# Reciprocals of the softmax through a table in DRAM instead of transposes: one fused attention and mixture-of-experts kernel

## The reference

```
B, H, S, D = 2, 8, 1152, 64
q_pool = q.reshape(B, H, S // 2, 2, D).mean(axis=3)            # 576 queries a head
scores = scale * q_pool @ k^T                                    # 576 x 1152
attn   = exp(scores - max(scores))
attn   = attn / (sum(attn) + 1e-9)                               # row by row
x      = attn @ v                                                # 576 x 64 a head
```

## Time and profile before

| | |
|---|---|
| median of 3 runs | 892.01 us |
| lowest and highest | 891.36, 893.62 us |
| the profiled execution | 892.18 us |
| its span | 890.2 us |
| mean granted clock of PE | 0.969 |
| attention, pairs 0 to 7 | about 20 to 270 us of the span |

### The profile page before, as it was taken

One profiled execution on the slowest core, in us unless ns is written; L12 is line 12 of the kernel. 1 busy time (PEld: TensorE's weight loads), 2 busy tenths in 40 slices (PEclk: granted clock), 3 DMA queues, 4 the chain that ended last, 5 costly groups with the idle time before them and its releaser, 6 DMA issues.

```text
span 890.2 us, 13115 instructions
## 1 busy us (share of the span) xinstructions
PE 837.6 (94%) x4706; PEld 714.4 (80%) x4707; DVE 397.0 (45%) x644; ACT 311.2 (35%) x509; POOL 218.1 (24%) x186
## 2 busy tenths in 40 slices
PE   6899999999999999999999999999996089999996
PEld 6787878788779898898989998898985078878885
DVE  3676766767575323421414223421414212796235
ACT  2565645556443211220303111220315012675233
POOL 4845955775631000000000000000000400232012
PEclk7999999999999999999999999999997579999998
DMA  7843425243263202200202002200000631596310
GB/s 186 266 112 93 107 68 134 67 111 90 70 183 120 71 1 95 95 1 1 94 1 94 0 0 94 95 1 1 1 1 0 226 105 47 192 331 227 144 42 19
DMA packets 30105, 79.83 MB, mean 90 GB/s; under 512 B 4007, under 2 KB 4007, under 8 KB 30064
## 3 DMA queue, kind: packets, MB, share of 16 engines
q1 hardware_dynamic: 26944, 69.99, 25.4%
q0 software_dynamic: 2960, 8.68, 2.8%
q10 hardware_dynamic: 160, 0.59, 0.3%
HBM read 69.52 MB, written 10.78 MB: 90 GB/s over the span
## 4 chain that ended last, share of the span: by engine, by line
PE 87%; DMA 4%; DVE 3%; POOL 2%; issue 2%; ACT 1%; SPq 0%; ACTq 0%; POOLq 0%; DVEq 0%
PE L L472 23%; PE L L415 22%; PE ring L388 8%; PE scores L353 8%; PE L L587 8%; PE L L561 7%; PE ring L367 6%; DMA rawQ<-in_qT 1%; DMA xr<-sorted_rows 1%; PE scores L376 1%; DVE negmax L785 1%; POOL sorted_rows L1146 1%; PE L L569 1%; ACT a L618 1%; DMA out<-o,destc 1%
## 5 line engine op out<-in xcount | busy, mean ns | idle before, releaser
L415 PE MATMUL L<-xTh,w1h 128*128 128x384 f32 x384 | 128.5, 335 | 0.0
L415 PE MATMUL L<-xTh,w1l 128*128 128x384 f32 x384 | 128.4, 334 | 0.0
L415 PE MATMUL L<-xTl,w1h 128*128 128x384 f32 x384 | 128.3, 334 | 0.0
L656 ACT ACTIVATE hh<-L 128x384 fp32r<-128x384 f32 x96 | 46.6, 491 | 201.3 <-PE L L415 201.3
L472 PE MATMUL L<-w2h,hh 128*128 128x512 f32 x288 | 114.3, 397 | 0.0
L472 PE MATMUL L<-w2h,hl 128*128 128x512 f32 x288 | 113.8, 395 | 0.0
L472 PE MATMUL L<-w2l,hh 128*128 128x512 f32 x288 | 113.7, 395 | 0.0
L1146 POOL DMA_INDIRECT sorted_rows<-acc,posi x9 | 10.7, 1188 | 414.3 <-DVE posi L976 411.9
L884 DVE SCALAR_TENSOR_TENSOR hl<-L,hh 128x384 fp32r<-128x384 f32 x96 | 52.9, 557 | 123.7 <-ACT hh L656 123.3
L618 ACT ACTIVATE a<-scores,negmax 128x1152 f32<-128x1152 f32 x72 | 88.0, 1222 | 39.6 <-DVE negmax L785 39.6
L785 DVE TENSOR_REDUCE negmax<-scores 128x1 f32<-128x1152 f32 x72 | 97.2, 1350 | 5.0 <-PE scores L353 4.8
(11 more groups left out here) (171 smaller groups left out, 1357.4 us busy)
## 6 DMA issues: line engine op xcount, KB each, us to landing
raw<-in_v SPq DMA_DIRECT2D x48, 512.0 KB, 5.5
raw<-in_w SPq DMA_DIRECT2D x32, 512.0 KB, 5.3
rawK<-in_kT SPq DMA_DIRECT2D x32, 288.0 KB, 4.5
rawQ<-in_qT SPq DMA_DIRECT2D x30, 288.0 KB, 5.7
sorted_rows<-filler SPq DMA_DIRECT2D x19, 257.0 KB, 5.7
V<-in_vr SPq DMA_DIRECT2D x16, 288.0 KB, 3.1
xr<-sorted_rows POOLq DMA_DIRECT2D x15, 257.0 KB
rawQ<-in_qT ACTq DMA_DIRECT2D x2, 288.0 KB, 6.1
```

The costliest lines, as they stand in the source:

```text
L415: last = pe.matmul(L1[i % L1_BANKS][:, 0:CW], w[:, d, wf], x[:, cols], start=(n == 0), stop=(n == 3 * DT - 1))
L656: act.activation(hh[c % 2][:, f, :], L1[i % L1_BANKS][:, 0:CW], ACT.Relu) \
```

## The change

PE no longer turns the reciprocals, and GpSimd no longer spreads them. SP does it by DMA (`share_rinv`): it waits for the reciprocals of a pair, stores the 128 x 9 numbers to a table `reciprocals` in DRAM, ordered by tile and query, waits until they have landed, and loads them back in three pieces, each row of queries repeated over 64 partitions, to a new tile `nb` of 128 x 576 in SBUF. The multiplication `y = o * nb` is one operation. In pairs 0 to 6 GpSimd does it, ahead of its split of the same pair: it prepares one of the next heads, multiplies and splits, and then prepares the other. In the last pair DVE does it. SyncE's share for pair j stands in its program between the loads for heads 2j + 4 and those for heads 2j + 5, and the last one ahead of the filler stores.

```diff
+            def share_rinv(j):
+                sp.wait_ge(S["rinv_ready"], j + 1)
+                sp.dma_start(recip[j].rearrange("(t p) -> p t", p=P), rinv[:].rearrange("p a t -> p (a t)")[:, 0:TPP],
+                             allow_slow_non_contiguous=True).then_inc(S["rinv_out"], 16)
+                sp.wait_ge(S["rinv_out"], 16 * (j + 1))
+                at_least(sp, S["y_ready"], j)
+                sp.dma_start(nb[0:DH, :], recip[j, 0:QS].partition_broadcast(DH)).then_inc(S["nb_in"], 16)
+                sp.dma_start(nb[DH:P, FULL * P:], recip[j, QS:QS + XW].partition_broadcast(DH)).then_inc(S["nb_in"], 16)
+                sp.dma_start(nb[DH:P, 0:FULL * P], recip[j, QS + XW:].partition_broadcast(DH)).then_inc(S["nb_in"], 16)
...
                 if n + 2 < NH:
                     load_kq(n + 2, n % 2)
+                if n % 2 == 0:
+                    share_rinv(n // 2 - 1)
+            share_rinv(PAIRS - 1)
...
                 if ahead:
                     score_part(g + LEAD, range(SC))
-                    spread_rinv(g, 0)
-                    spread_rinv(g, 2)
...
             times_v(PAIRS - 1, 1)
-            pe.wait_ge(S["spread_ready"], 2 * PAIRS)
-            for t in range(FULL):
-                last = pe.transpose(L2[1][:, t * P:(t + 1) * P], spread[:, t * P:(t + 1) * P], ident[:])
-            last.then_inc(S["nb_ready"], N_DONE - 1)
-            pe.transpose(L2[0][:, 0:P], spread[:, FULL * P:], ident[:]).then_inc(S["nb_ready"], 1)
...
                 if s == 0:
-                    at_least(act, S["y_ready"], Y_DONE * j)
+                    at_least(act, S["y_ready"], j)
...
                     take_last(g - 1)
-                    if spread_blocks(g - 1):
-                        normalize(g - 1)
...
+            dve.wait_ge(S["nb_in"], 48 * PAIRS)
+            dve.wait_ge(S["x_lo"], PAIRS - 1)
+            tt_(y[:], o[:], nb[:], ALU.mult).then_inc(S["y_ready"], 1)
...
             def split_x(j):
-                pool.wait_ge(S["y_ready"], Y_DONE * (j + 1))
+                pool.wait_ge(S["o_low"], v_done(j, 1))
+                pool.wait_ge(S["o_high"], v_done(j, 1))
+                pool.wait_ge(S["nb_in"], 48 * (j + 1))
+                at_least(pool, S["x_lo"], j)
+                pool.tensor_tensor(y[:], o[:], nb[:], ALU.mult).then_inc(S["y_ready"], 1)
+                pool.wait_ge(S["y_ready"], j + 1)
...
             for j in range(PAIRS):
-                if j:
-                    spread_pair(j - 1)
...
-            spread_pair(PAIRS - 1)
```

More of the change, by code:

```diff
@@ L29 @@
 V_STEP = (5, TPP)
-N_STEP = {2: ((0, 0), (1, 2)), 3: ((2, 0), (3, 2)), 4: ((FULL, 0),)}
 WARM = 23
-Y_DONE = 4
-N_DONE = sum(len(blocks) for blocks in N_STEP.values())
 SC = 3
@@ L56, with attention_moe_moe_kernel @@
 NEPS = 1e-6
-def attention_moe_moe_kernel(nc, kT, qT, vr, dom, w1, w2, emb, tau, v1, v2, rows, out):
+def attention_moe_moe_kernel(nc, kT, qT, vr, dom, w1, w2, emb, tau, v1, v2, rows, recip, out):
     ctx = ExitStack()
@@ L122, in attention_moe_moe_kernel @@
         totale = sb("totale", [P, TPP + 1], F32, att)
-        spread = sb("spread", [P, (FULL + 1) * P], F32, att)
+        nb = sb("nb", [P, QS], F32, att)
         rinv = sb("rinv", [P, 2, FULL + 1], F32, att)
@@ L248, in last_view @@
             return halved(g % TPP, spare(g + LEAD, 1).rearrange("p (i q) -> p i q", q=P))
-        def spread_blocks(g):
-            j, k = g // TPP, g % TPP
-            return N_STEP[k] if j and k in N_STEP else ()
         names = """consts_in kq_in0 kq_in1 v_in0 v_in1 k_hi k_lo q_sum q_scaled q_hi q_lo s_ready max_ready
-            exp_ready den_ready rinv_ready t_ready0 t_ready1 t_ready2 nb_ready a_out0 a_out1 a_out2 o_ready o_low o_high spread_ready y_ready pads_ready emb_in
+            exp_ready den_ready rinv_ready t_ready0 t_ready1 t_ready2 nb_in a_out0 a_out1 a_out2 o_ready o_low o_high rinv_out y_ready pads_ready emb_in
             x_hi x_lo w1_hi w1_lo w2_hi w2_lo l1_ready h_hi l1_free l2_ready l2_free
@@ L391, in times_v @@
                 last.then_inc(S["o_ready"], 1)
[L393 to L399, removed]
             def up_tile(e, c, f):
@@ L800, in take_o @@
                 if s == 0:
-                    at_least(dve, S["y_ready"], Y_DONE * j)
+                    at_least(dve, S["y_ready"], j)
                 dve.tensor_copy(o[s * DH:(s + 1) * DH, HALF:QS], bank(("V", j, s))[DH:P, 0:HALF]) \
@@ L811, in rinv_pair @@
                     .then_inc(S["rinv_ready"], 1)
[L813 to L838, removed]
             dve.wait_ge(S["kq_in0"], 64)
@@ L868, in _ @@
             take_o(PAIRS - 1, 1)
[L869 to L873, removed]
+            dve.wait_ge(S["o_low"], NH)
+            dve.wait_ge(S["o_high"], NH)
+            dve.wait_ge(S["nb_in"], 48 * PAIRS)
+            dve.wait_ge(S["x_lo"], PAIRS - 1)
+            tt_(y[:], o[:], nb[:], ALU.mult).then_inc(S["y_ready"], 1)
             last_cols = slice((PAIRS - 1) * QS, PAIRS * QS)
-            dve.wait_ge(S["y_ready"], Y_DONE * PAIRS)
+            dve.wait_ge(S["y_ready"], PAIRS)
             dve.tensor_copy(xTh[:, last_cols], y[:]).then_inc(S["x_hi"], 1)
@@ L1075, in prep_q @@
                     .then_inc(S["q_lo"], 1)
[L1077 to L1084, removed]
-            def split_x(j):
-                pool.wait_ge(S["y_ready"], Y_DONE * (j + 1))
+            def split_x(j):
+                pool.wait_ge(S["o_low"], v_done(j, 1))
[4 more added lines that the diff above has]
+                pool.wait_ge(S["y_ready"], j + 1)
                 cols = slice(j * QS, (j + 1) * QS)
@@ L1204 @@
     rows = nc.dram_tensor("sorted_rows", ((SLOTS + 2) * P, ROW), F32, kind="Internal").ap()
+    recip = nc.dram_tensor("reciprocals", (PAIRS, TPP * P), F32, kind="Internal").ap()
     out = nc.dram_tensor("out_0", (N, D), F32, kind="ExternalOutput").ap()
-    attention_moe_moe_kernel(nc, *aps, rows, out)
+    attention_moe_moe_kernel(nc, *aps, rows, recip, out)
     r = run_bass_kernel_spmd(nc, [feed], core_ids=[0])
```

## The result

The changed kernel takes **897.12 us** (median of 5 runs, 895.73 to 898.29), the one before 892.01 us (median of 5 runs here, 891.16 to 893.62): a ratio of 1.0055, with a 95% interval of 1.0037 to 1.0073. The forecast was 889.0 us, in a range of 887.6 to 892.0. The kernel became 5.1 us slower where 3.0 us less were forecast; time and range were both wrong. The profiled execution took 896.78 us. Of the 21 runs of the kernel before that stand beside the first four experiments, one took 2151.69 us; it counts in no ratio.

A forecast was written before the change was run, and what follows sets the result against it. PE's chain, and what makes PE wait, was taken to bound the kernel. Gains of 2.5 us (pairs 1 to 7) and 0.5 us (last transposes), other terms 0, took 892.01 to 889.0 us, range 887.6 to 892.0.

The forecast's parts named there:

- Step 1, the pairs: Pairs 1 to 7 lose the transposes and DVE's `y`: 0.36 us a pair, 2.5 us in all.
- The control, pair 0: Pair 0 runs tiles 2 to 5 without transposes and `y`: 6.90 us, against 7.26 us in pair 4.
- DVE alone is the limit: Rival, chance 0.07: DVE alone limits the pairs, each gains 1.1 us, and the time is 883.8 us.
- Step 2, the five transposes: The last pair's five transposes on PE, between V and the next up tile, go: 0.5 us gained.
- Step 3, DVE's last `y` and what hangs on it: Last pair: `y` (0.8 us with gap) through `hl` takes 2.65 us; reciprocals may take 9.1 us at no cost.
- The allowance: Last pair: from the reciprocals computed at 262.7 to their latest landing at no cost, 271.8: 9.1 us.
- Step 4, the way through DRAM: Storing the reciprocals to DRAM takes 3.0 us, loading them back 3.6; with hand-overs 6.9 us, inside the 9.1.
- The upper end: Way through DRAM if each 4 B element costs 0.12 us: write 10.4, way 14.3, stall 5.2 us.
- The last round trip is late: Rival, chance 0.17: beyond 9.1 us PE stalls at the fifth up tile; a 14.3 us way gives 894.2 us.
- Steps 5 and 6: GpSimd's `y` (1.43 us) fits its slack in each pair, and SyncE's queue delays nothing needed: both cost 0.

The follow-up runs named there:

- the first four experiments: Four edits of the changed kernel: last pair's reciprocals by PE, 888.97 us; `hl` before last multiplication, 888.8; store in 36 B runs, 887.94; 50 idle matmul calls, 899.62.
- the probes: Test stores of varied shape after each pair's loads, added to the changed kernel with `hl` ahead of the last multiplication; they took 2.3 to 11.4 us.

## Why the prediction was wrong

- **Step 1, the pairs: right.** 2.25 us between the reciprocals of pair 0 and those of pair 7 (0.32 a pair), where 2.5 were forecast; the 2.68 us at the first up tile come nearer to it by the luck of an earlier start. The control, pair 0, was the right row. That PE's issue and DVE were both "close to the limit" is now narrower: DVE's `y` was all of it. In this the rival "DVE alone is the limit" had the right engine and the wrong price: taking 1.1 us off DVE gave 0.32 us a pair.
- **Step 2, the five transposes: right,** 0.52 us.
- **Step 3, DVE's last `y` and what hangs on it: right.** `y` took 0.76 us and the fifth up tile began 2.69 us after its start, against 2.65 + 0.1. The allowance was 9.1 us, and 14.7 - 5.66 = 9.0 came out.
- **Step 4, the way through DRAM: the step that failed.** It took 14.7 us, from 260.0 to 274.7, where 6.9 were forecast. Of the 7.8 us between, 7.3 are the store, 10.3 us for 3.0. The packets were priced rightly, 1.4 us forecast and about 1 seen; what was wrong is the 1.6 us of latency, carried over from the load of V into SBUF. Here the landing came 8 us after the last packet. The rest is the loads, 4.3 us from the first issue to the last landing instead of 3.6: an issue held the queue for 0.45 to 0.60 us instead of 0.34, and the last load took 3.2 us to land instead of 2.7. That the store's form is the cause is shown (1.5 us in runs of 36 B, and no loss); what makes elements side by side land late stays open.
- **The upper end was right by accident.** Its 10.4 us is what came, but from 0.12 us for each element, and the store's time hardly grows with the elements. The choice between the ends was taken by the pace of packets, which wasn't what decided. Trace and the Trainium skill ("DMA: Bandwidth & Descriptors", Anatomy of one DMA) agree in one thing: it puts most of a DMA's fixed time behind the last byte, in the target's receipt, with HBM the slowest. Its size, about 2 us, which it gives for DMAs issued by GpSimd, is near the stores of 36 B runs (1.5 to 2.4 us, issued by SP), not the 8.5 to 10.3 us of this one, in which 8 us pass behind the last packet. The same page (Specifications) names 512 B as the size below which the engines read, modify and write; here all of the probes are below it, and those 16 B apart took 3.2 us, so that rule alone doesn't divide the fast from the slow.
- **The rival had the mechanism and not the whole price.** "The last round trip is late" had a chance of 0.17 and 894.2 us. With the measured 14.7 us it gives 892.0 + 5.6 - 3.0 = 894.6. The missing 2.7 us are the clock after the stall, which stood in no term: I charged a wait on PE one for one, though nothing had shown what the clock does behind a pause. With it the sum is 897.3, and 897.12 was measured.
- **Steps 5 and 6: right.** GpSimd's `y` takes 1.40 us and starts at 159.27 in pair 4; it is done 2.6 us before `o` is taken. The stores of pairs 1 to 6 took 8.5 to 9.4 us and the loads of V and K/Q went 4 to 5 us later behind their pair's reciprocals than before, and nobody waited for them.

## What to carry to other kernels

Price a round trip through DRAM from a store of the same form, small and scattered as it is; where no row shows one, give the upper end as much weight as the lower, and ask at which place the waiting engine has other work to do first: moving `hl` ahead of the wait turned 5 us of loss into 3 us of gain, with no byte moved faster. Count a stall on PE as its length plus what the clock costs behind it. Which engine limits a ring is told by putting the removed work back on one at a time, since their busy shares (99 and 70%) pointed at the wrong one here.

## What the hardware showed that I had not expected

- A store of 4.5 KB to DRAM took 1.5 us in runs of 36 B, about 3 us as single 4 B elements 16 B or more apart, and 8.3 to 11.1 us as single elements side by side, with the packets gone in about 1 us. Even 128 or 144 such elements took 7.4 and 7.0 us.
- In the kernels with single elements and without a test store, the table's store of the last pair was slower than those of pairs 1 to 6: 10.0 to 10.6 us against 8.3 to 9.4 to SP's next issue; pair 0 had 9.6 to 9.8. The one with 25 idle calls, on a chip of its own, had 11.1, 9.1 to 9.4 and 10.6 us. Why isn't known.
- After a pause of 5.5 us PE ran at a granted clock of 0.50 for 5.6 us, after one of 2.25 us, behind 5.7 us of matmuls, for 3.2 us, beginning 1.4 us after it had started again; that cost 2.7 and 1.5 us.
- The three loads that spread a row over 64 partitions held SP's queue for 0.45, 0.60 and 0.60 us, in single cases for 1.3 to 2.7. A load of V holds it for 0.34 us, but for 0.58 right behind these, so the spreading itself isn't shown to be the cause.
